# Attention, mixture of experts and feed-forward on one core: another order around steps 0 and 1, and another order of TensorE's work in the first sequence's slots

## What is computed

```python
# attention: a window of 15 neighbours on each side, plus 24 block summaries
k_sum = k.reshape(B, H, nb, block, D).max(axis=3)      # block 32
v_sum = v.reshape(B, H, nb, block, D).mean(axis=3)
scores_all = concat([where(|i - j| < 16, scale * q @ k.T, -1e9), scale * q @ k_sum.T + log(32)])
x = softmax(scores_all) @ concat([v, v_sum])
# experts: 4 of them, each on all 1536 tokens, 512 -> 1024 -> 512
p = domain_probs / sum(domain_probs)
x = sum over e of p[:, e] * (relu(x @ w1[e]) @ w2[e])
# feed-forward: 512 -> 2048 -> 512
h = x @ w_in
out = (h * sigmoid(1.702 * h)) @ w_out
```

## Time and profile before

| | before |
|---|---|
| median of 3 runs | 846.4 us |
| the profiled execution | 844.88 us |
| its span | 843.1 us |
| TensorE busy | 818.5 us (97%) |
| VectorE, ScalarE, GpSimd busy | 537.9, 399.4, 553.3 us |
| chain that ended last, TensorE's share | 91% |
| mean granted clock of TensorE | 0.988 |

### The profile page before, as it was taken

How to read it: one execution, slowest core, us unless ns; L and a number is a source line. 1 busy time by engine, 2 the same in 40 slices (tenths; PEclk the granted TensorE clock), 3 DMA queues, 4 the chain that set the end, 5 groups by cost and what they waited for, 6 DMA issues and landing times.

```text
span 843.1 us, 13848 instructions
## 1 busy us (share of the span) xinstructions
PE 818.5 (97%) x5014; PEld 804.2 (95%) x5014; DVE 537.9 (64%) x1194; ACT 399.4 (47%) x859; POOL 553.3 (66%) x412
## 2 busy tenths in 40 slices
PE   5888999999999999999999999999999999999998
PEld 4677999999999999999999999999999999999998
DVE  6867666656665566566566666666676665665665
ACT  3764544544444454434334344444455555454541
POOL 3667566656566699756556578877578887466450
PEclk9988999999999999999999999999999999999999
DMA  9992116141112112212113112112113122322102
GB/s 268 277 214 97 51 58 213 51 150 71 51 66 104 51 51 98 72 51 103 67 51 113 58 51 101 51 53 98 51 51 101 50 58 93 125 69 83 51 1 76
DMA packets 26420, 74.72 MB, mean 89 GB/s; under 512 B 14704, under 2 KB 15856, under 8 KB 20208
## 3 DMA queue, kind: packets, MB, share of 16 engines
q1 hardware_dynamic: 26352, 73.84, 27.3%
HBM read 70.66 MB, written 3.17 MB: 88 GB/s over the span
## 4 chain that ended last, share of the span: by engine, by line
PE 91%; SPq 2%; DMA 2%; issue 2%; DVE 1%; POOL 1%; ACT 0%; DVEq 0%; ACTq 0%; POOLq 0%
PE bank L1115 30%; PE bank L1117 29%; PE bank L1116 29%; DMA k_win<-k_w 2%; PE bank L1070 1%; PE bank L1107 1%; PE bank L1081 1%; SPq L402 1%; SPq L409 0%; POOL xb_other_lo L548 0%; SPq L415 0%; POOL prob L498 0%; DVE masked L858 0%; DVE row_sum_e L868 0%; DVE bank L959 0%
## 5 line engine op out<-in xcount | busy, mean ns | idle before, releaser
L926 DVE TENSOR_TENSOR xa<-bank,xa 128x384 f32<-128x384 f32 x352 | 195.8, 557 | 219.9 <-PE bank L1117 215.5
L1115 PE MATMUL bank<-h_hi,wd_hi 128*128 128x384 f32 x768 | 257.3, 335 | 1.6 <-DVE h_lo L970 1.4
L1117 PE MATMUL bank<-h_lo,wd_hi 128*128 128x384 f32 x768 | 256.9, 334 | 0.0
L1116 PE MATMUL bank<-h_hi,wd_lo 128*128 128x384 f32 x768 | 256.8, 334 | 0.0
L541 POOL TENSOR_TENSOR wd_lo<-stage,wd_hi 128x1024 fp32r<-128x1024 f32 x48 | 114.9, 2393 | 162.0 <-ACT wd_hi L694 162.0
L735 ACT ACTIVATE h_hi<-bank 128x384 fp32r<-128x384 f32 x192 | 94.5, 492 | 229.5 <-DVE bank L959 182.1
L1115 PEld LDWEIGHTS bank<-h_hi,wd_hi 128*128 128x128 f32 x768 | 144.4, 188 | 3.0 <-issue 3.0
L1116 PEld LDWEIGHTS bank<-h_hi,wd_lo 128*128 128x128 f32 x768 | 144.3, 188 | 0.0
L1117 PEld LDWEIGHTS bank<-h_lo,wd_hi 128*128 128x128 f32 x768 | 144.3, 188 | 0.0
L529 POOL TENSOR_TENSOR wu_lo<-stage,wu_hi 128x1024 fp32r<-128x1024 f32 x48 | 115.0, 2396 | 3.9 <-ACT wu_hi L682 3.9
L1115 PE MATMUL bank<-xb_other_hi,wu_hi 128*128 128x384 f32 x336 | 112.3, 334 | 0.3 <-ACT snap L719 0.3
(11 more groups left out here) (77 smaller groups left out, 1271.8 us busy)
## 6 DMA issues: line engine op xcount, KB each, us to landing
stage<-weights SPq DMA_DIRECT2D x48, 1024.0 KB, 4.8
k_win<-k_w SPq DMA_DIRECT2D x8, 720.0 KB, 8.6
v_win<-v_w SPq DMA_DIRECT2D x8, 576.0 KB, 9.1
q_bd<-q_t SPq DMA_DIRECT2D x16, 192.0 KB, 9.0
p_bc<-p_rows SPq DMA_DIRECT2D x8, 384.0 KB, 4.8
v_cols<-v_t SPq DMA_DIRECT2D x6, 384.0 KB, 5.9
out<-xa SPq DMA_DIRECT2D x4, 384.0 KB, 7.8
out<-xa SPq DMA_DIRECT2D x8, 192.0 KB, 1.9
```

The costliest lines, as they stand in the source:

```text
L926: nc.vector.tensor_tensor(at, y_bank(g, t), at, ALU.add).then_inc(y_taken, 1)
L1115: nc.tensor.matmul(dst, w_h, a_h, start=first, stop=False, skip_group_check=True)
L1116: nc.tensor.matmul(dst, w_l, a_h, start=False, stop=False, skip_group_check=True)
L1117: return nc.tensor.matmul(dst, w_h, a_l, start=False, stop=last, skip_group_check=True)
```

## The change

- **Loads.** The weights of step 0 are loaded after the keys and queries of unit 3, not before them.
- **Low parts of step 0's weights.** GpSimd makes them in four halves (`low_first`) in slots 11, 12, 14 and 15, not in two whole ones in slots 10 and 11; ScalarE's `high_raw(0)` moves from slot 9 to 10 and `high_down(0, .)` from slot 10 to 13.
- **Spreads.** `spread_value_means` of units 1 to 3 comes one slot later (behind the next group's `normalize`). Unit 4's key maxima are formed in slot 15 and spread behind `sum_weights(1)`; they were formed behind `low_moved(3)` and spread behind `low_sums(1)`.
- **Slots.** TensorE takes values, sums of values, transposes, scores in each slot; it took scores, transposes, values, sums. All first tiles of step 0 come behind the last values; the first halves of C11 and C21 stood between them.
- **Banks.** Tile C22 of step 0 lies in bank 7 and not in bank 0, so P1 of step 1, which writes bank 0, waits for the last masking and not for C22's low part.
- **Step 1.** TensorE has P1, P2, scores, P5 and then the first down tile; before it was P1, down 0, scores, P2, down 1, P5. ScalarE has `high_sums(1)` right behind `high_raw(1)`, and `high_down(1, .)`, `high_moved(0, 4)` and `exponent(12)` between `keep(1, 0)` and `high_raw(2)`. VectorE's order is another one too, and unit 4's `value_sums` moves behind `take_y(0, 3)`.

```diff
 (sync)
-            load_weights(0)
             load_keys(3)
             load_queries(3)
+            load_weights(0)
 (gpsimd, slots)
-                    else:
+                for u in unit_starting(slot, L_MEAN + 2):
+                    if u:
                         spread_value_means(u, norm_done, slot - L_NORM + 1)
-                if slot == 10:
-                    low_raw(0)
-                if slot == 11:
-                    low_down(0)
+                if slot in (11, 12):
+                    low_first(slot - 11)
+                if slot in (14, 15):
+                    low_first(slot - 12)
 (gpsimd, steps)
                     sum_weights(g + 1)
+                    if g == 0:
+                        spread_key_maxima(KT)
                     low_raw(g + 1)
 (scalar)
             high_moved(0, 1)
             high_raw(1)
+            high_sums(1)
             high_hidden(0, "C12")
             high_hidden(0, "C22")
-            high_moved(0, 3)
             high_hidden(0, "C11")
             high_hidden(0, "C21")
-            high_moved(0, 4)
-            high_sums(1)
-            high_down(1, 0)
-            high_down(1, 1)
+            high_moved(0, 3)
...
                 keep(g, 0)
+                if g == 1:
+                    high_moved(0, 4)
+                    high_down(1, 0)
+                    high_down(1, 1)
+                    exponent(B_GROUPS)
                 if more:
                     high_raw(g + 1)
 (vector, step 1)
+                    add_c11(1)
+                    mask_scores(B_GROUPS)
+                    gate(1, "C11")
+                    take_y(0, 0)
+                    low_moved(4)
+                    low_hidden(1, "C11")
+                    take_y(0, 1)
+                    invert_sums(B_GROUPS)
+                    take_y(0, 2)
+                    low_moved(5)
+                    take_y(0, 3)
+                    value_sums(KT)
 (tensor)
-                for k in group(slot, L_SCORE):
-                    scores(k)
-                for k in group(slot, L_TRANS):
-                    transpose(k)
                 for k in group(slot, L_VAL):
                     values(k)
                 for u in unit_starting(slot, L_MEAN):
                     turn_value_sums(u)
...
+                for k in group(slot, L_TRANS):
+                    transpose(k)
+                for k in group(slot, L_SCORE):
+                    scores(k)
...
+            product(1, "P1")
+            product(1, "P2")
+            scores(B_GROUPS)
+            product(1, "P5")
+            down(0, 0)
+            product(1, "P6")
+            down(0, 1)
+            product(1, "P7")
+            down(0, 2)
+            down(0, 3)
+            turn_value_sums(KT)
+            down(0, 4)
+            down(0, 5)
+            transpose(B_GROUPS)
+            product(1, "P4")
+            down(0, 6)
+            product(1, "P3")
+            down(0, 7)
```

More of the change, by code:

```diff
@@ L746, in _ @@
                     value_means(u)
-                if slot == 9:
+                if slot == 10:
                     high_raw(0)
-                if slot == 10:
-                    high_down(0, 0)
-                    high_down(0, 1)
                 if slot == 12:
@@ L755, in _ @@
                     high_moved(0, B12)
+                    high_down(0, 0)
+                    high_down(0, 1)
                 if slot == 16:
@@ L781, in _ @@
                 for k in step_group(g):
-                    exponent(k)
+                    if g > 1:
+                        exponent(k)
                 for k in step_group(g - 1):
@@ L990, in _ @@
                     normalize_weights()
+                if slot == 13:
+                    low_moved(0)
                 if slot == 14:
-                    low_moved(0)
                     low_moved(B12)
+                    sum_first(1)
                 if slot == 15:
-                    sum_first(1)
+                    key_maxima(KT)
             low_moved(6)
@@ L1001, in _ @@
             low_hidden(0, "C12")
-            sum_first(2)
             low_hidden(0, "C22")
@@ L1005, in _ @@
             gate(0, "C21")
-            sum_first(3)
+            sum_first(2)
             low_hidden(0, "C11")
             low_hidden(0, "C21")
+            sum_first(3)
             low_moved(3)
-            key_maxima(KT)
             sum_first(4)
             for g in range(1, STEPS):
-                take_y(g - 1, 0)
-                if g > 1:
-                    low_hidden(g - 1, "C12")
[L1017 to L1020, removed]
-                add_c11(g)
-                take_y(g - 1, 1)
-                gate(g, "C11")
-                take_y(g - 1, 2)
-                low_hidden(g, "C11")
-                if g == 1:
-                    low_moved(4)
-                take_y(g - 1, 3)
-                for k in step_group(g):
-                    invert_sums(k)
-                if g == 1:
-                    low_moved(5)
+                if g == 1:
+                    add_c11(1)
[10 more added lines that the diff above has]
+                    value_sums(KT)
+                else:
+                    take_y(g - 1, 0)
+                    low_hidden(g - 1, "C12")
+                    for k in step_group(g):
+                        mask_scores(k)
+                    add_c11(g)
+                    take_y(g - 1, 1)
+                    gate(g, "C11")
+                    take_y(g - 1, 2)
+                    low_hidden(g, "C11")
+                    take_y(g - 1, 3)
+                    for k in step_group(g):
+                        invert_sums(k)
                 take_y(g - 1, 4)
@@ L1129, in product @@
                         pe.wait_ge(x_done, ALL_GROUPS)
-                    else:
-                        before = g - 2 if g > ATT_OVER + 2 else g - 1
-                        pe.wait_ge(hlo_done, ready(before, "C21" if before else "C22"))
+                    elif g == 1:
+                        pe.wait_ge(masked_done, B_GROUPS)
+                    else:
+                        pe.wait_ge(hlo_done, ready(g - 2 if g > ATT_OVER + 2 else g - 1, "C21"))
                 elif name == "P2":
@@ L1217, in _ @@
             first_tile("C21", 1, True)
-            for g in range(1, STEPS):
+            product(1, "P1")
[16 more added lines that the diff above has]
+            down(0, 7)
+            for g in range(2, STEPS):
                 product(g, "P1")
```

41 lines of the change are left out of this document (27 added, 14 removed).

## The result

The changed kernel is slower. Its median is 849.32 us (847.57 to 853.60, 20 runs) against 844.45 us (841.93 to 848.81, 20 runs) for the kernel before; the ratio is 1.0055, with a 95% interval of 1.0041 to 1.0068. The prediction said 846.4 us and gave 0.74 to no change that can be told; the time is 2.9 us above that, and the change itself is +4.9 us where +0.8 was worked out. The measured time lies in the range, near its upper end.

What follows compares the result with a forecast made beforehand. TensorE, busy 818.5 of 843.1 us, was taken as the bound. A gain of 1.1 us up to M and a loss of 1.9 from M to N gave +0.8; between 845.7 and 847.2 it said 846.4 us, range 840 to 850.5.

Steps and rivals of the forecast that it cites:

- M: End of step 0's last first-tile matmul on TensorE; 61.98 us before, forecast 60.9, 1.1 us gained.
- N: Start of step 2 on TensorE, 86.68 us before; nothing after it was expected to change.
- N - M: TensorE's stretch through step 1: 17.1 work, 4.3 and 1.9 waits, 3.3 clock, 26.6 us against 24.7.
- P7's wait: TensorE in step 1 stands 4.3 us for ScalarE's copy `keep(1, 1)`, queued behind `high_raw(2)`, which waits for GpSimd.
- the wait of the turned sums: TensorE in step 1 waits 1.9 us (1.5 to 2.4) for VectorE's `value_sums(4)`, placed behind `take_y(0, 3)`.
- V: Start of `value_sums(3)` on VectorE, 37.77 us before; forecast 35.7, when unit 3's value columns land.
- the term from the spread to M: TensorE's last values, transposes and copies, 6.8 us at the lower clock, then first tiles, 8.35 us without a wait.
- Values first: TensorE's slot order: scores of groups 7 to 11 reached about a microsecond later than they could be.
- (b): Rival: clock falls near 37, spread ends at 48.0, M 63.1, first part gains nothing; +3.0, 847.9 us; chance 0.18.
- (c): Rival: TensorE's clock falls again behind the turned sums, 2.2 us on top of (b); +5.2, 850.1 us; chance 0.12.
- (a): Rival: everything covered, M at 59.0, P7 waiting 1 us at most; -6.4, 838.5 us; chance 0.14.
- The rule on the port: VectorE and GpSimd exclude each other for whole instructions; `low_moved(0)` would delay unit 3's spread from 45.9 to 46.4.

Runs made afterwards that it cites:

- m_raw: Changed kernel with ScalarE's `high_raw(2)` in step 1 moved behind the copy that P7 waits for and `high_moved(0, 5)`; ratio to the kernel before 1.0046.
- m_vsum: Changed kernel with VectorE's value sums of unit 4 in step 1 moved ahead of `take_y(0, 0)`; one run, 847.9 us.
- u_step: Changed kernel with step 1's orders on TensorE, ScalarE and VectorE undone; ratio to the kernel before 1.0022.
- loads_only: Kernel before with one edit: step 0's weights loaded after the keys and queries of unit 3; ratio 0.9980.
- u_spread: Changed kernel with the spread of value means of units 1 to 3 one slot earlier again, values still first; ratio to the kernel before 1.0033.
- x_warm: Changed kernel plus 24 matmuls nobody reads, behind the transposes of groups 9, 10 and 11; ratio to the kernel before 1.0041.
- best2: best1 with `low_moved(4)` moved directly behind `add_c11(1)` and `low_moved(0)` back in slot 14 on VectorE; ratio to the kernel before 0.9932.
- best3b: best2 with `low_moved(4)` one instruction earlier on VectorE, ahead of `sum_first(4)`; ratio to the kernel before 0.9926.
- best1: Changed kernel with scores first, spread early, and step 1 reordered on ScalarE and VectorE; 838.62 us, ratio to the kernel before 0.9927.

## Why the prediction was wrong, step by step

**What was right.** Only M and N count: span - N never moved. N - M was forecast at 26.6 us and measured at 26.6 and 26.3. P7's wait was forecast at 4.3 us by ScalarE's copy behind GpSimd's sums and measured at 4.7; the wait of the turned sums was forecast at 1.9 us and measured at 1.5; the clock fell behind the first (0.50 from 80 to 86) and not again behind the second. With 17.1 us of work that leaves 3.3 us for the clock and the restarts, which is the price given; 18 matmuls at 0.32 us in place of 0.17 are 2.6 us of it. m_raw, m_vsum and u_step show both waits to be what they were called. In the first part VectorE waited at `value_sums(3)` for the value columns, by 2.0 and 1.35 us, and unit 3's spread was what `values(9)` waited for. From V to the end of the spread the schedule gave 45.9 - 35.7 = 10.2 us, and the profiles have 10.5 and 11.4. The keys of unit 3 did not land near 29 in these two executions: VectorE's key maxima begin at 33.5 and 31.2. In loads_only, u_spread, m_raw, m_vsum, x_warm, best2 and best3b, whose loads came sooner, they begin at 28.9 to 29.8.

**What was wrong: the term from the spread to M.** It was put at 6.8 us at the lower clock plus 8.35 us of first tiles, 15.15 in all; it measures 18.0 and 17.25. The mechanism was right, values, transposes and copy by turns at the lower clock. The size was not, and the part that failed is the first tiles: the prediction took the stretch of 7 us of the earlier trace rows as the pattern and let them run at the upper clock, in 8.35 us. They took 10.9 and 10.2 us; the attention's part took 7.1 us both times, for 6.8. Measured, the lower clock lasts from 49 to 63, through the first 15 of the 48 first-tile matmuls (in the second profile through ten). Before, TensorE worked without a gap from 47.94 on and had the upper level back at about 53; here gaps of 0.78 and 0.69 us lie between its pieces (the rows above), the last ends at 56.83, and the upper level is back at about 62.8. That the short gaps delayed it is my reading of these rows. x_warm fills them and the long wait ahead of them and takes 13.6 us, close to the 13.05 that the prediction has for the upper clock.

**The sum again.** M - V was forecast at 60.9 - 35.7 = 25.2 and is 28.5: 3.3 us too little, of which 2.1 to 2.9 are the term above and the rest the way to the spread. The forecast total of +0.8 plus 3.3 is +4.1; the medians say +4.9. Term by term, forecast and found: M - V +1.0 and +4.4, N - M +1.9 and +1.8, and the earlier V that the loads bring -2.1 and -1.3. This last is worked out as the remainder, and loads_only (-1.1 by medians) agrees with it inside a wide interval; it is where the 0.8 us between +4.1 and +4.9 would lie.

**The undercosted edit.** "Values first" was costed as about a microsecond at each of some groups, hidden behind VectorE, and the late spread as something beside it. Undoing the order in the changed kernel shows 4.9 us, undoing the spread 3.0 us, and the order alone costs 0.8 to 1.9 us. The low parts in halves and the move to bank 7 have no run of their own; with the scores first, all edits ahead of M together leave M - V at 23.6 us, against 23.1 with the loads alone. The prediction named the queue behind `values(6)` and `values(9)` and let it cost only its own wait.

**The rivals.** (b), the first part gives nothing, gave 847.9 us; it put the loss on one more fall of the clock near 37. In the changed kernel's first profile the clock stayed at 1.00 there, in the second it fell, and M - V was the same in both (28.5 and 28.65): what both have is the long stretch from 49 on. (c) was the nearest in time (850.1), by luck, as it had the wrong place: no second fall came behind the turned sums. (a) did not come near; best1 shows that it asked for another order on ScalarE and VectorE. The load of step 3's weights, issued near 89 instead of 73.5, cost nothing: there is no wait for it in step 2 or 3.

**The rule on the port.** What the prediction took from the Trainium skill, page "SBUF — State Buffer", section "Who interferes with whom", agrees with the trace: `low_moved(0)` began at 48.18, and the spread, begun at 48.70 beside it, took 2.08 us and not 1.47, for the half microsecond given. The kernels with the spread early have 1.46 or 1.47 again.

## What to carry to other kernels

On an engine that works in order, the position of an instruction is judged by what it waits for: putting at the head of a slot the one instruction whose operand was just made later turned an edit that cost nothing and one that cost 0.8 to 1.9 us into 4.9 us. A wait that is forecast should be priced with what follows it on TensorE: here the work behind it came in pieces with gaps, and the lower clock reached 5 us into the dense work behind them; with the idle time filled it did not fall. And when a wait has been traced to one instruction on another engine, look at the second to last thing that is late before expecting all of it back; with P7's wait for the copy out of the way, m_raw, best1, best2 and best3b each had another of 1.5 to 3.8 us in step 1.

## What the runs showed of the hardware

- TensorE busy for 10.49 of 14 us, in pieces, stayed at a granted clock of 0.51 (the lower level, 1.2 GHz) from 49 to 63 us. With the idle time filled by matmuls that nobody reads, up to one gap of 1.3 us, the same stretch had 1.00 (x_warm, 46 to 62). A wait of 1.82 us was followed by the lower level in the second profile of the changed kernel and not in the first.
- A VectorE instruction with both inputs in SBUF, 0.95 us by itself, took 2.99 us (m_raw), 3.05 us (best2) and 2.75 us (best3b) when a GpSimd instruction of 2.35 to 2.4 us had begun 0.1 to 0.5 us before it. It is not shared but waited out: in best2 GpSimd ends at 66.33 and VectorE 0.8 us later. The other way round, GpSimd's low part took 2.99 instead of 2.39 us. The tensor reduction of value sums took 0.94 or 0.95 us in each place.
- The same load, with the same bytes ahead, landed up to 5.5 us apart between executions of nearly the same program (V from 34.8 to 40.4 on one and the same chip: loads_only and u_step). A single profile's M says little without its V.
